# Fused rotary attention and two feed-forward layers: value products of chunk 0 with 64-column operands that add up in one half of the rows

## The reference

```python
q_rot, k_rot = (rotate(q), rotate(k))
scores = scale * np.matmul(q_rot, k_rot.transpose(0, 1, 3, 2))
scores = scores - np.max(scores, axis=-1, keepdims=True)
attn = np.exp(scores)
attn = attn / (np.sum(attn, axis=-1, keepdims=True) + 1e-09)
attn_out = np.matmul(attn, v)
x = attn_out.transpose(0, 2, 1, 3).reshape(B * S, H * D)
h = x @ moe_w_in;   x = (h * (1.0 / (1.0 + np.exp(-h)))) @ moe_w_out
h = x @ moe2_w_in;  y = (np.where(h > 0.0, h, np.exp(np.minimum(h, 0.0)) - 1.0)) @ moe2_w_out
```

## Time and profile before

| what | value |
|---|---|
| median of 3 runs | 555.92 us (555.57 to 557.42) |
| the profiled execution | 555.34 us, its span 553.5 us |
| TensorE busy | 530.0 us, 96% of the span |
| VectorE, ScalarE, GpSimd busy | 282.9, 344.3, 347.6 us (51%, 62%, 63%) |
| the chain that ended last | 87% of it TensorE, 68% of it line L1032 |

### The profile page before, as it was taken

How to read it: one execution, slowest core, us unless ns; L and a number is a source line. 1 busy time by engine, 2 the same in 40 slices (tenths; PEclk the granted TensorE clock), 3 DMA queues, 4 the chain that set the end, 5 groups by cost and what they waited for, 6 DMA issues and landing times.

```text
span 553.5 us, 9215 instructions
## 1 busy us (share of the span) xinstructions
PE 530.0 (96%) x3228; PEld 522.8 (94%) x3228; DVE 282.9 (51%) x515; ACT 344.3 (62%) x726; POOL 347.6 (63%) x285
## 2 busy tenths in 40 slices
PE   1878899999999999999999999999999999999997
PEld 1777899999999999999999999999999999999997
DVE  5788865643368953446653337883234440067400
ACT  3899887755477856557774557775455653366531
POOL 5998989769637646645654654444454665656662
PEclk9999999999999999999999999999999999999999
DMA  8776655656455355344343333333434343444440
GB/s 319 212 222 189 168 185 140 187 186 184 128 155 182 120 167 165 109 131 135 118 125 123 118 110 102 117 117 116 123 98 123 124 134 124 133 115 133 134 143 28
DMA packets 45788, 79.50 MB, mean 144 GB/s; under 512 B 6832, under 2 KB 14384, under 8 KB 45744
## 3 DMA queue, kind: packets, MB, share of 16 engines
q1 hardware_dynamic: 44016, 76.57, 45.5%
q10 hardware_dynamic: 1728, 2.36, 1.2%
HBM read 63.57 MB, written 2.36 MB: 119 GB/s over the span
## 4 chain that ended last, share of the span: by engine, by line
PE 87%; ACT 3%; POOL 3%; DVE 2%; DMA 2%; issue 2%; SPq 0%; ACTq 0%; DVEq 0%
PE banks L1032 68%; PE banks L962 5%; PE banks L998 4%; PE banks L942 3%; PE banks L948 3%; PE banks L991 2%; ACT prob L521 2%; POOL w_lo L403 1%; PE banks L973 1%; DVE neg_max L698 1%; DMA k_raw<-k 1%; DMA w_raw<-w 1%; PE banks L1010 1%; POOL k_raw L358 1%; PE banks L1000 0%
## 5 line engine op out<-in xcount | busy, mean ns | idle before, releaser
L403 POOL TENSOR_TENSOR w_lo<-w_raw,w_hi 128x512 fp32r<-128x512 f32 x192 | 247.2, 1290 | 187.9 <-ACT w_hi L564 187.6
L564 ACT CAST w_hi<-w_raw 128x512 fp32r<-128x512 f32 x189 | 117.7, 624 | 47.1 <-PE banks L1032 42.0
L1032 PE MATMUL banks<-x_lo,w_hi 128*128 128x384 f32 x384 | 129.5, 337 | 0.5 <-DVE g_lo L787 0.5
L1032 PE MATMUL banks<-g_lo,w_hi 128*128 128x384 f32 x384 | 128.9, 336 | 0.0
L1032 PE MATMUL banks<-x_hi,w_lo 128*128 128x384 f32 x384 | 128.6, 335 | 0.0
L1032 PE MATMUL banks<-g_hi,w_lo 128*128 128x384 f32 x384 | 128.5, 335 | 0.0
L1032 PE MATMUL banks<-x_hi,w_hi 128*128 128x384 f32 x384 | 128.4, 334 | 0.0
L1032 PE MATMUL banks<-g_hi,w_hi 128*128 128x384 f32 x384 | 128.4, 334 | 0.0
L698 DVE TENSOR_REDUCE neg_max<-banks 128x1 f32<-128x576 f32 x72 | 54.2, 753 | 63.9 <-PE banks L948 63.1
L576 ACT ACTIVATE act_buf<-banks 128x384 f32<-128x384 f32 x96 | 47.4, 494 | 54.7 <-PE banks L1032 54.2
L1032 PEld LDWEIGHTS banks<-x_lo,w_hi 128*128 128x128 f32 x384 | 72.1, 188 | 1.9 <-issue 1.0
(11 more groups left out here) (83 smaller groups left out, 670.4 us busy)
## 6 DMA issues: line engine op xcount, KB each, us to landing
w_raw<-w SPq DMA_DIRECT2D x192, 256.0 KB, 2.7
q_raw<-q SPq DMA_DIRECT2D x11, 384.0 KB, 4.5
q_one<-q_raw SPq DMA_DIRECT2D x44, 96.0 KB, 2.5
k_raw<-k SPq DMA_DIRECT2D x7, 576.0 KB, 4.8
k_st<-k_raw SPq DMA_DIRECT2D x28, 144.0 KB, 2.5
v_raw<-v SPq DMA_DIRECT2D x8, 320.0 KB, 3.9
out<-act_buf ACTq DMA_DIRECT2D x12, 192.0 KB, 2.8
k_both<-k_st SPq DMA_DIRECT2D x15, 144.0 KB, 2.9
```

The source lines that it names most:

```text
L403: nc.gpsimd.tensor_tensor(w_st[LO][:, slot, :], w_raw[:, slot, :], w_st[HI][:, slot, :].bitcast(F32), ALU.subtract).then_inc(w_lo_done, 1)
L564: nc.scalar.copy(w_st[HI][:, slot, :], w_raw[:, slot, :]).then_inc(w_hi_done, 1)
L1032: last = nc.tensor.matmul(dst, w_st[wp][:, slot, m * P:(m + 1) * P], src[xp][:, tile, :], start=start and n == 0, stop=stop and n == 2)
```

## The change

For heads 0 to 6 of chunk 0 the value products take 64-column operands: for each of the four full blocks of tokens hi*lo, lo*hi and hi*hi, and for the last block two, so fourteen products of 384 moving columns. All of them add up in rows 0 to 63 of the one bank. They are cut in three groups (blocks 0 and 1; blocks 2 and 3; the last) that stand in the three tiles of the next head. The result of an even head is copied by ScalarE (`copy_out_lo`), that of an odd head by VectorE (`copy_out`), and nothing is added. Since each head's first product overwrites the bank, it waits for the copy of the head before (`out_lo_copied`). The widening, spreading and scaling of a pair move in the loops, the spread sums of pairs 0 to 2 go to the bank of the ends, and GpSimd multiplies both halves of the keys (all those of chunk 0 and of head pair 4, r = 5 included) and of the queries (r up to 3) in one instruction. Head 7 and chunks 1 and 2 keep their products.

```diff
 def inv_rows(p):
-    return banks[:, 4 if p % 4 == 3 else PV_BANK, 0:CT]
+    return banks[:, 4 if p % 4 == 3 else END_BANK if p < 3 else PV_BANK, 0:CT]
...
+def keys_products(r):
+    raw = k_raw[r % 2]
+    pool.wait_ge(k_in[r % 2], 16 * (r // 2 + 1))
+    pool.wait_ge(k_table_in, 16)
+    nc.gpsimd.tensor_tensor(raw[:, :, :], raw[:, :, :], k_table[:, :, :], ALU.mult).then_inc(k_scaled, 2)
...
@@ ScalarE, copy_out_lo @@
-                if i // H == 1:
+                if i < DIRECT:
+                    nc.scalar.copy(dst, pv_out[lower, :]).then_inc(out_lo_copied, 1)
+                elif i // H == 1:
...
@@ ScalarE, the loop @@
-                if t == 0 and i >= 2:
+                if t == 0 and i >= 2 and i % 2 == 0:
                     copy_out_lo(i - 2)
...
                     if t == 2:
                         values_hi(p)
+                        if p:
+                            widen_sums(p - 1)
                 elif p:
-                    if t == 0:
-                        widen_sums(p - 1)
...
@@ VectorE @@
+            def copy_out(i):
+                p = i // 2
+                dve.wait_ge(pv_done, i + 1)
+                if p >= 2:
+                    dve.wait_ge(x_lo_done, p - 1)
+                nc.vector.tensor_copy(head_out[p % 2][upper, :], pv_out[lower, :]).then_inc(out_lo_copied, 1)
...
@@ VectorE, the loop @@
                 if n < H * QN - 1:
                     max_tile(n + 1)
+                if i % 2 and t == 1 and p:
+                    scale_outputs(p - 1)
                 if n:
                     probs_lo(n - 1)
                 if t == 0 and i:
                     end_lo(i - 1)
-                if t == 0 and i >= 2:
-                    add_outputs(i - 2)
+                if i % 2 and t == 0 and p:
+                    copy_out(i - 2)
...
@@ TensorE, transpose_end @@
+                if t == 0 and i in (3, 5, 7):
+                    pe.wait_ge(out_scaled, i // 2)
...
+            def direct_products(i, tiles):
+                buf, rows = buffer_of(i), pv_out[lower, :]
+                if tiles[0] == 0:
+                    pe.wait_ge(pt_lo_done, QN * i + QN)
+                    pe.wait_ge(v_lo_done, i // 2 + 1)
+                    if i:
+                        pe.wait_ge(out_lo_copied, i)
+                for m in tiles:
+                    if m == 4:
+                        pe.wait_ge(end_lo_done, i + 1)
+                        for part in (LO, HI):
+                            last = nc.tensor.matmul(rows, v_st[:, i, m, value_cols(i, part)], pt_end[buf], start=False,
+                                                    stop=part == HI)
+                        last.then_inc(pv_done, 1)
+                    else:
+                        for part, probs in ((HI, LO), (LO, HI), (HI, HI)):
+                            nc.tensor.matmul(rows, v_st[:, i, m, value_cols(i, part)], pt[probs][buf][:, m, :],
+                                             start=m == 0 and probs == LO, stop=False)
...
@@ TensorE, the loop @@
+                if t == 0 and i:
+                    direct_products(i - 1, range(2))
+                if t == 0 and i % 2 and i > 2:
+                    spread_sums(i // 2 - 1)
                 if t == 1:
                     transpose_end(n - 1)
                 if t >= 1:
                     transpose_end(n)
-                if t == 1 and i % 2 and i > 2:
-                    spread_sums(i // 2 - 1)
-                if t == 1 + i % 2 and i:
-                    value_products(i - 1)
+                if t == 1 and i:
+                    direct_products(i - 1, range(2, 4))
+                if t == 2 and i:
+                    direct_products(i - 1, range(4, VT))
```

More of the change, by code:

```diff
@@ L98, in inv_rows, with added, value_cols @@
         def inv_rows(p):
-            return banks[:, 4 if p % 4 == 3 else PV_BANK, 0:CT]
+            return banks[:, 4 if p % 4 == 3 else END_BANK if p < 3 else PV_BANK, 0:CT]
+        def added(i):
+            return i + 1 - DIRECT
+        def value_cols(i, part):
+            return (lower, upper)[(i + part) % 2]
         def scores(n):
@@ L375, in queries_times, with queries_products @@
                 nc.gpsimd.tensor_tensor(raw, raw, query_table(n, r // 4), ALU.mult).then_inc(q_scaled, 1)
+            def queries_products(r):
+                raw = q_raw[r % 2]
+                pool.wait_ge(q_in[r % 2], 16 * (r // 2 + 1))
+                nc.gpsimd.tensor_tensor(raw[:, :, :], raw[:, :, :], table[:, :, 0:CT], ALU.mult).then_inc(q_scaled, 2)
             def queries_add(r):
@@ L420, in rope_queries @@
             def rope_queries(r):
-                queries_times(r, 0)
-                queries_times(r, 1)
+                if r < 4:
+                    queries_products(r)
+                else:
+                    queries_times(r, 0)
+                    queries_times(r, 1)
                 queries_add(r)
-            def rope_keys(r):
-                keys_times(r, 0)
-                keys_times(r, 1)
-                keys_add(r)
             rope_queries(1)
-            rope_keys(1)
+            keys_products(1)
+            keys_add(1)
             queries_lo(1)
@@ L446, in _ @@
             rope_queries(5)
-            rope_keys(5)
+            keys_products(5)
+            keys_add(5)
             for n in range(ALL_UNITS):
@@ L740, in scale_outputs @@
                 dve.wait_ge(row_done, p + 1)
-                dve.wait_ge(out_added, 2 * p + 2)
+                if p < 3:
+                    dve.wait_ge(out_lo_copied, 2 * p + 2)
+                else:
+                    dve.wait_ge(out_added, added(2 * p + 1))
                 nc.vector.tensor_tensor(head_out[p % 2][:, :], head_out[p % 2][:, :], inv_rows(p), ALU.mult) \
@@ L839, in _ @@
                     end_lo(i - 1)
-                if t == 0 and i >= 2:
-                    add_outputs(i - 2)
+                if i % 2 and t == 0 and p:
+                    copy_out(i - 2)
                 if i % 2 == 0:
-                    if t == 1 and p:
+                    if t == 0 and p:
                         invert_sums(p - 1)
                 else:
-                    if t == 1 and p:
-                        scale_outputs(p - 1)
                     if t == 2 and p and i < H - 1:
@@ L981, in value_products @@
                     pe.wait_ge(v_lo_done, i // 2 + 1)
-                if i % 2:
-                    pe.wait_ge(out_added, i)
-                elif i:
+                if i == DIRECT:
+                    pe.wait_ge(out_lo_copied, i)
+                elif i % 2:
+                    pe.wait_ge(out_added, added(i - 1))
+                else:
                     pe.wait_ge(out_scaled, i // 2)
```

12 lines of the change are left out of this document (8 added, 4 removed).

## The result

| what | before | after |
|---|---|---|
| median of 16 runs each | 555.77 us | 558.08 us (557.47 to 558.99) |
| the profiled execution, its span | 555.34, 553.5 us | 558.32, 556.5 us |
| TensorE, VectorE, ScalarE, GpSimd busy | 530.0, 282.9, 344.3, 347.6 us | 535.9, 282.8, 343.0, 345.8 us |

The ratio is 1.0042 (95% interval 1.0036 to 1.0049): slower by 2.3 us, where 1.8 was forecast. No run here compares TensorE's format (fp32r) with another, so that it is the faster one is not shown.

What follows compares the result with a forecast made beforehand. In the head stage ScalarE and VectorE set the pace and TensorE follows. Head terms of +1.4 to +1.5 and the end put head 7's value products +1.8 us later, carried through to 557.7 us (range 553.6 to 561.5).

Steps and rivals of the forecast that it cites:

- Odd heads: Heads 3, 5, 7: first group waits for VectorE's copy behind both lo parts; 6.80 us against 6.71, +0.1.
- Even heads: Heads 2, 4, 6: ScalarE takes over the widening, delaying the next exponential; 6.35 becomes 6.77 us.
- shared access to memory: GpSimd's joined multiplication could take more than two apart; with 1.2 of 13 us to spare, not visible in the time.
- the 0.42: Time the widening holds ScalarE before the next exponential in each even head, counted fully on the path: +0.42 us.
- Heads 1 and 2 taken as even: Heads 1 and 2 lose the lump of nine products before their next transposes and gain the groups; no net change counted.
- POOL's joined multiplications: GpSimd's keys and queries: joining saves 0.34 us per pair of heads, but GpSimd waits for ScalarE, so nothing counted.
- The end: End of head stage: tile 23's transposes at 65.24 and head 7's value products at 68.0 us, against 66.21 before.
- The sum: Head stage: three even heads and heads 3 and 5 add 1.4 to 1.5 us at head 7's first exponential.
- Lumps were the cost: Rival, chance 0.2: copy ready by the scores' end at +2.1, copies and a lump of products saved; 553.2 us.
- Drains: Rival, chance 0.17: TensorE drains 0.16 us at each of some 20 operand switches, 3.3 us more; 561.0 us.
- Nothing either way: Rival, chance 0.2: widening finds a gap or copy is shorter than the addition, and the end cancels; 555.9 us.

Runs made afterwards that it cites:

- copy-earlier run: Changed kernel with VectorE's copy_out in odd heads placed ahead of the two lo parts, not behind them; median 555.40 us, ratio 0.9988 to the kernel before.
- POOL's wait: Changed kernel with GpSimd's key addition for head pairs 3 and 4 made to wait until VectorE's split is done; median 556.84 us, ratio 1.0020.
- split earlier: Changed kernel with VectorE's split of a finished pair moved ahead of the third tile's lo part in odd heads; median 556.90 us, ratio 1.0018.
- widening back: Changed kernel with ScalarE's widening of a pair's sums returned to the first tile of the odd head; median 557.76 us, ratio 1.0032.
- tile 23 first: Changed kernel with the second group of head 6's value products behind tile 23's transposes, not ahead of them; median 558.15 us, ratio 1.0040.

## Why the prediction was right, and where it was off

**Odd heads: right.** Forecast 6.80, measured 6.82 and 6.83. By terms, in head 5 (start 45.57): the first group at +3.36 where +3.20 was forecast; the group 1.09 (1.13); spreading to scaling 0.52 (0.53); to the lo part 0.47 (0.47); lo part 0.60 (0.68); maximum and exponential 0.79 (0.79). The lo parts and the copy came as walked; the 0.16 is the way from the copy's end (48.78) to TensorE's start (48.93), 0.15, where I had put 0.02. TensorE stood still 1.27 and 1.28 ahead of the group, forecast 1.1. The copy-earlier run shows the reason itself: without that wait odd heads last 6.08.

**Even heads: the step that failed.** "6.35 becomes 6.77" was right for what it counted: 6.77 and 6.78 wherever the split was short. It left out that the odd head's new order puts the split of the pair onto POOL's key addition, 0.9 us in head 4 and 1.0 in head 6, of which 0.5 and 0.6 reached the end of the head: late maximum, late lo part, TensorE's first group 0.49 and 0.66 late, late exponential (0.38 and 0.52). The prediction had named the shared access to memory, but only as something that would slow POOL, whose time is hidden; VectorE's side of it was on the path. A row of before hinted at it: the split took 0.74 where another operation of 128x384 took 0.55. In head 2, which has no split, the head grew by only 0.2, though the widening's own part there is 0.41 (6.89, and 6.48 with it back).

**What the 0.42 is.** It says where the next exponential falls. It is not a cost of its own in a pair: the prediction took nothing off in the odd heads for the widening's leaving, but with the copy early a pair lasts 12.9 us wherever the widening stands (6.77 and 6.08, or 6.45 and 6.47). With the copy late, going back won 0.3 us in all. The sum of 0.42 for each of three even heads is right for the heads of this kernel and wrong as the price of this one move.

**Heads 1 and 2 taken as even.** In the profiled execution head 1 grew from 5.09 to 5.71, 0.6 us. In the other runs with the change's products it was 5.15 to 5.55, and 5.16 where TensorE had its fast pace in time (last section). So 0.1 is the change's, about 0.5 belongs to that execution, and this is most of what the traces differ by more than the medians.

**POOL's joined multiplications: right at nothing** in the stage. Two joined cost 2.67 where two apart cost 2.81: 0.14 saved, forecast 0.17. The cost at the end that a joined one can have showed in other runs.

**The end.** Tile 23's transposes to head 7's products were forecast 2.76 apart and were 2.90. The transposes came at 66.77 for 65.24; nearly all of that is carried in from the heads.

**The sum.** Head 7 began 2.96 us later than before, where +1.46 was forecast: +0.6 from head 1, +1.1 from heads 4 and 6, -0.2 from head 2. Head 7's products: +3.46. TensorE had next to no gap from there on and kept it, but for the 0.5 of the wait at 104 us, which before has and after has not; that leaves the 3.0 of the spans.

**How much of the nearness is luck.** 558.08 against 557.7 looks closer than the working was. The prediction lacked POOL's hold on the split, worth 1.2 us. Against it stand two things that it lacked as well: head 2 grew by 0.2 less than forecast, and after is spared the wait at 104 us, 0.5. The way it was forecast by, odd heads held by the copy, is right; the even heads' part of the number is not.

**The rivals.** *Lumps were the cost*: its condition failed, the copy was not ready at +2.1; yet with the copy earlier it came true in part, 555.40 and not 553.2, so the kernel won 0.4 to 0.6 us in all and not 2.7. What held it there is, by the trace, TensorE, busy 25.0 of 26.1 us in that run. *Drains*: the run with 128-column operands rules out that they cost what was priced, here. The Trainium skill ("TensorEngine Tiling (Array Packing)", Key Properties) has a drain at each change of mode; between 128*128 and 128*64 no row shows one, and the measurement decides. *Nothing either way*: ruled out by the interval of the ratio, though the margin of 0.3% is near. *The chances*: the working puts somewhat less than a third of its own forecast below 557.6, but its middle, 557.7, lies only 0.1 above that line, so nearly half should have stood there: of the 0.43 some 0.2 for no change, and 0.4 and not 0.47 for slower. The 0.3% margin there is also wider than what 16 runs each told apart (1.0036 to 1.0049).

**How 2.3 us are made up**, by the medians: POOL's hold on the split 1.2 (558.08 to 556.84, the run with POOL's wait); the copy behind the lo parts 1.4 (556.84 to 555.40; by the ratios, each to before on its own chip, 1.8); less the gain of 0.4 to 0.6 that the edit brings with its copy in the right place. The first is shown by an edit that does nothing else. The second is the difference of two runs, in both of which the hold is gone from the middle of the stage.

## What to carry to other kernels

An instruction that costs 0.55 us in one place can cost 1.4 to 2.5 in another, if it has both inputs in SBUF and GpSimd is in a long instruction: when a change shifts VectorE against GpSimd, list such instructions and see what GpSimd is doing at their new times. A result that another engine waits for belongs ahead of work that nobody waits for, in the queue of the engine that makes it; one copy moved up two places was worth 2.7 us here (558.08 to 555.40), of which 1.2 came because it also moved the split away from GpSimd's addition. And an added wait on an engine with time to spare can be a gain. Last, look where the limit goes when a wait is gone: here, by the traces, it went to TensorE, to which the change itself had given more products.

## What the runs showed of the hardware that was not expected

**The hold goes by whole instructions.** The split ended 0.40 to 0.42 us behind the end of POOL's instruction, whatever that was (an addition of 1.43 or a multiplication of 2.67), while alone it takes 0.55. What was in progress when the split began had to end first; the split then needed 0.4 more. So joining two instructions of POOL, which saves 0.14 us, makes the longest possible stall longer by nearly the other's length: 2.37 and 2.51 were seen.

**TensorE's start in head 1 varies.** The rows of the scores, by the distance of starts, show the pace of TensorE. Before:

```profile
17.42 0.44 PE L942 MATMUL banks<-k_st,q_one 128*128 128x288 f32 x1
17.66 0.44 PE L948 MATMUL banks<-k_st,q_two 128*128 128x288 f32 x1
...
18.32 0.69 PE L962 MATMUL banks<-ident,prob 128*128 128x128 f32 x4
...
19.11 0.29 PE L942 MATMUL banks<-k_st,q_one 128*128 128x288 f32 x1
19.24 0.29 PE L948 MATMUL banks<-k_st,q_two 128*128 128x288 f32 x1
```

After:

```profile
18.27 1.06 PE L997 MATMUL banks<-ident,prob 128*128 128x128 f32 x4
...
19.37 0.44 PE L983 MATMUL banks<-k_st,q_two 128*128 128x288 f32 x1
19.61 0.36 PE L977 MATMUL banks<-k_st,q_one 128*128 128x288 f32 x1
19.81 0.29 PE L983 MATMUL banks<-k_st,q_two 128*128 128x288 f32 x1
```

A product of 288 columns took 0.24 us at first, the pace of 1.2 GHz, and 0.13 later, near the 0.12 of 2.4 GHz. Before had changed to the fast pace by 18.98; after was still slow at 19.37 and changed at 19.6. The granted clock's column prints 1.00 for all these stretches, so only the starts tell. From the first transpose of that tile to its fourth score product it is 0.92 us in before (18.32 to 19.24) and 1.54 in after (18.27 to 19.81), which is the 0.6 by which head 1 grew. The other runs with the change's products bear it out: the distance is 1.41, 1.27, 1.13 and 0.83 us in the runs with the split earlier, POOL's wait, the widening back and tile 23 first, and their heads 1 last 5.55, 5.45, 5.32 and 5.16. These have head 1 in the same order, so it is the execution that differs and not the kernel. This is why a shift of a few tenths has to be read from medians and not from two profiled executions.
